# Where ScalarE makes the masks and the exponentials of a softmax round: masks ahead of the second turned tile, exponentials ahead of the last copy

## Time and profile before

| what | value |
|---|---|
| three runs | 974.4, 969.75, 970.98 us; median 970.98 |
| profiled execution | 970.57 us, span 969.0 us, granted clock 0.99 |
| TensorE busy | 908.8 us, 94% |
| VectorE busy | 717.8 us, 74% |
| GpSimd busy | 660.3 us, 68% |
| ScalarE busy | 577.4 us, 60% |
| chain that ended last | TensorE 71%, issue 10%, ScalarE 6%, VectorE 5%, GpSimd 3% |

### The profile page before, as it was taken

How to read it: one execution, slowest core, us unless ns; L and a number is a source line. 1 busy time by engine, 2 the same in 40 slices (tenths; PEclk the granted TensorE clock), 3 DMA queues, 4 the chain that set the end, 5 groups by cost and what they waited for, 6 DMA issues and landing times.

```text
span 969.0 us, 17781 instructions
## 1 busy us (share of the span) xinstructions
PE 908.8 (94%) x5132; PEld 690.2 (71%) x5133; DVE 717.8 (74%) x2191; ACT 577.4 (60%) x1226; POOL 660.3 (68%) x624
## 2 busy tenths in 40 slices
PE   4688999999999999999999999999999999999996
PEld 2354857768585776758586685957685998998895
DVE  5999999989999989999999899999503621251120
ACT  2577786777777777767777677776523321342211
POOL 7999997887988789888878879885453312231221
PEclk9999998999999999999999999999999999999998
DMA  5821121232211222121112222111043061116110
GB/s 196 253 58 46 42 59 57 58 113 55 60 44 56 68 58 67 44 68 51 49 58 57 63 58 60 53 30 46 13 145 100 18 221 56 54 38 222 43 54 32
DMA packets 69270, 70.84 MB, mean 73 GB/s; under 512 B 15456, under 2 KB 50560, under 8 KB 69184
## 3 DMA queue, kind: packets, MB, share of 16 engines
q1 hardware_dynamic: 65264, 59.44, 20.2%
q0 software_dynamic: 3920, 10.40, 3.5%
HBM read 59.05 MB, written 10.76 MB: 72 GB/s over the span
## 4 chain that ended last, share of the span: by engine, by line
PE 71%; issue 10%; ACT 6%; DVE 5%; POOL 3%; DMA 1%; POOLq 0%; SPq 0%; DVEq 0%; ACTq 0%
PE m_ps L1385 17%; PE m_ps L1467 10%; PE s_ps L1450 8%; PE t_ps L1342 7%; PE m_ps L1411 7%; PE o_ps L1358 5%; PE m_ps L1399 5%; PE s_ps L1324 4%; PE s_ps L1329 3%; PE o_ps L1450 3%; DVE top L1130 2%; ACT probs L927 1%; POOL dispatch_list L395 1%; PE m_ps L1418 1%; PE m_ps L1404 1%
## 5 line engine op out<-in xcount | busy, mean ns | idle before, releaser
L787 POOL TENSOR_TENSOR scores<-scores,below 128x576 f32<-128x576 f32 x144 | 200.3, 1417 | 88.0 <-ACT below L919 87.4
L1385 PE MATMUL m_ps<-xT,w_sb 128*128 128x192 f32 x1152 | 199.6, 331 | 1.2 <-ACT xT L963 1.2
L1385 PEld LDWEIGHTS m_ps<-xT,w_sb 128*128 128x128 f32 x1152 | 189.8, 193 | 1.5 <-ACT xT L963 1.5
L1130 DVE MAX8 top<-upper 128x8 f32<-128x288 f32 x384 | 159.4, 448 | 0.7 <-issue 0.6
L1132 DVE MATCH_REPLACE8 upper<-top,upper 128x288 f32<-128x288 f32 x288 | 125.3, 443 | 0.2 <-issue 0.2
L1342 PEld LDWEIGHTS t_ps<-ident,probs 128*128 128x128 f32 x720 | 80.3, 142 | 59.6 <-issue 51.1
L927 ACT ACTIVATE probs<-scores,shift 128x576 f32<-128x576 f32 x144 | 111.3, 783 | 18.3 <-issue 18.3
L956 ACT COPY probsT<-t_ps 128x640 f32<-128x640 f32 x192 | 103.4, 564 | 28.0 <-PE t_ps L1342 26.8
L1342 PE MATMUL t_ps<-ident,probs 128*128 128x128 f32 x720 | 107.4, 280 | 11.8 <-ACT probsT L956 11.8
L795 POOL TENSOR_SCALAR probs<-probs,inverse 128x576 f32<-128x576 f32 x144 | 105.4, 754 | 7.3 <-DVE inverse L1120 7.2
L919 ACT ACTIVATE below<-scores,steep_kth 128x576 f32<-128x576 f32 x144 | 106.6, 771 | 2.2
(11 more groups left out here) (208 smaller groups left out, 1789.1 us busy)
## 6 DMA issues: line engine op xcount, KB each, us to landing
k_sb<-keys_t SPq DMA_DIRECT2D x48, 288.0 KB, 2.6
v_sb<-values SPq DMA_DIRECT2D x48, 256.0 KB, 2.7
raw<-e_w SPq DMA_DIRECT2D x12, 1024.0 KB, 5.4
maxout_rows<-x_rows SPq DMA_DIRECT2D x18, 256.0 KB, 2.2
q_sb<-queries_t SPq DMA_DIRECT2D x48, 64.0 KB, 2.5
w_sb<-w SPq DMA_DIRECT2D x2, 1536.0 KB, 8.3
q_rest<-queries_t SPq DMA_DIRECT2D x96, 16.0 KB, 2.3
v_sb<-values SPq DMA_DIRECT2D x48, 32.0 KB, 2.6
```

Of the source, the lines that this page charges most:

```text
L787: nc.gpsimd.tensor_tensor(scores[:, r % RING, i, :], scores[:, r % RING, i, :], below[:, i, :], ALU.subtract).then_inc(masked_ready, 1)
L1130: nc.vector.max(best, src).then_inc(topk_step, 1)
L1385: ins = nc.tensor.matmul(dst[:, a * BLK:(a + 1) * BLK], w_sb[:, w, c, (first + a) * P:(first + a + 1) * P], xT[:, m % 2, c, b % SPAN * BLK ...
```

## The change

Only the places of ScalarE's steps change. `scalars` and all three `under` of round r stand at a new place, 5, ahead of H1 of round r. `exp(0)` and `exp(1)` of round r stand at place 9, ahead of the last M of round r. `exp(2)` of round r stands after Q0 of round r+1. Nothing is added or removed.

```diff
-AFTER_Q0, AFTER_H0, AFTER_H2, AHEAD_OF_LAST = 0, 3, 7, 9
+AFTER_Q0, AHEAD_OF_H1, AFTER_H2, AHEAD_OF_LAST = 0, 5, 7, 9
...
                 if in_range(r - 1):
-                    under_2, exp_0, exp_1, exp_2 = softmax_steps(r - 1)[3:]
-                    steps += [(AFTER_Q0, under_2), (AFTER_Q0, exp_0), (AFTER_H0, exp_1), (AFTER_H0, exp_2)]
+                    steps.append((AFTER_Q0, softmax_steps(r - 1)[6]))
+                if in_range(r):
+                    steps += [(AHEAD_OF_H1, step) for step in softmax_steps(r)[:4]]
...
                 if in_range(r):
-
-                    steps += [(AHEAD_OF_LAST, step) for step in softmax_steps(r)[:3]]
+                    steps += [(AHEAD_OF_LAST, step) for step in softmax_steps(r)[4:6]]
```

## The result

| kernel | runs | median | ratio to before | profiled execution | span | mean clock |
|---|---|---|---|---|---|---|
| before | 4 | 970.51 us | | 970.57 | 969.0 | 0.99 |
| changed | 4 | 1092.58 us (1087.77 to 1098.51) | 1.125, 95% interval [1.119, 1.132] | 1092.48 | 1090.9 | 0.956 |

What follows compares the result with a forecast made beforehand. The prediction took TensorE to set the pace, held up by waits for ScalarE's copies. To 970.6 us it added 91.2 of waits and 10 for the clock, giving 1071.8 us, stated as 1072, with a range of 1042 to 1112.

Steps and rivals of the forecast that it cites:

- TensorE sets the pace, and H1's copy is what it needs.: Masks ahead of H1's copy make TensorE's H2 start 2.24 us later in most rounds, 2.41 in parts 3 and 7.
- The exponentials ahead of the last copy.: Ahead of the last M copy: later copies make Q1 after parts 1 and 3 wait longer, +0.2 us per cycle.
- exp(2) early brings nothing but kth in time.: After the next round's Q0: VectorE's 1.08 us waits go without a gain in time, and kth comes sooner.
- `full_sum` with almost no wait: Sign on VectorE: its waits for the exponentials, 26.7 us in 25 rounds before, nearly vanish.
- Rival C: VectorE's kth comes too late for ScalarE, which stands with H1's copy; +42 us, 1114 us; chance 0.07.
- The first rounds.: Rounds 0 to 5: exponentials at the round's end hold back the next Q0 copy; +16.0 us at round 6.
- All waits.: Whole kernel: 16.0 to round 6, 12.7 in rounds 6 to 13, 58.0 in four cycles, 4.5 at the end; 91.2 us.
- The clock: From T of part 3 to L of part 4: a fall in all six cycles, four more than before, +10 us.
- I count none there: At the 2.24 us H2 waits of the A rounds: no clock falls, as a 0.87 us wait there had none.
- Rival A: The clock falls at A rounds' H2 waits too, in every second round; +45 us for the clock, 1107 us; chance 0.15.
- the main theory: Whole kernel: longer TensorE waits plus four more clock falls, 1072 us; chance 0.62.
- D, faster.: VectorE sets the pace, H2's wait vanishes in TensorE's slack and sums come sooner; 951 us; chance 0.03.

Runs made afterwards that it cites:

- experiment 3: The changed kernel with the masks one item later, behind H1's copy instead of ahead of it; 999.31 us, ratio 1.034 to before.
- Experiment 1: The changed kernel with four unused products filling TensorE's wait ahead of H2 wherever the first half does not end with Y; 1054.54 us, ratio 1.091 to before.
- experiment 2: The kernel before with only scalars and masks moved ahead of H1, the three exponentials left in their old places; 1123.76 us, ratio 1.161.
- experiments 4 and 5: The changed kernel with softmax rounds 0 to 5 in the old order, 1074.17 us; the same plus masks behind H1's copy, 984.04 us.
- experiments 6 and 7: The changed kernel with scalars and one mask, then two masks, ahead of H1's copy and the others behind it; 1011.19 us, then 1034.91 us.
- experiment 10: The kernel before: scalars, masks ahead of second half's first M; part 3's mask 1 after next Q0; part 2's last exponential behind H1's copy; 960.30 us.
- experiments 8 and 9: The kernel before with scalars and masks 0 and 1 ahead of the second half's first M, not its last, on two visits; 962.88 and 967.35 us.

## Why the prediction was right, and where it was short

- *TensorE sets the pace, and H1's copy is what it needs.* Right; experiment 3 shows it alone. The price was put at 2.24 us and is 2.16 (a wait of 2.07 in the timeline): from H1's copy to H2 it takes 0.81 us (383.52 to 384.33), not the 0.89 of the earlier trace rows. The waits in parts 3 and 7 are 2.17 (forecast 2.41), part 6 none. Part 2 waits 2.01 at H2, with the 0.42 at H1 gone, so it costs 0.6 more than before; forecast 0.5.
- *The exponentials ahead of the last copy.* Their own cost was forecast at +0.2 per cycle. Experiment 1, where the clock does not fall, shows Q1 waiting 0.45 and 0.72 us per cycle where it was 0.61 and 0.89: the change gives back 0.3 us here. (In the changed kernel itself the second of them is hidden, as V ran at the lower clock.)
- *exp(2) early brings nothing but kth in time.* Two things in this were wrong. The prediction let `full_sum` go earlier and named "`full_sum` with almost no wait" as a sign; it waits 132.6 us in place of 26.7, in nearly every round. In round 23 it stands for 4.14 us until exp(2) is done, behind a Q0 copy that comes later:

```profile
391.51 0.16 DVE L1115 TENSOR_REDUCE full_sum<-sums 128x3 f32<-128x6 f32 x1 [4.14 <-ACT probs L927]
```

VectorE has no more work than before, and the longer rounds leave it idle at this place. As TensorE sets the pace, this costs nothing. And "nothing" was too little: experiment 2 shows that with the exponentials left behind `kth` is late and the loss 35 us larger. Rival C was a real threat, which the other half of the change takes away. How the two halves hang together was in the prediction only as half a sentence.
- *The first rounds.* Forecast 16.0 us at Q1 of round 6. It stands at 114.22 in place of 97.16, 17.1 later, and Q2 of the same round at 121.26 in place of 105.70, 15.6 later. In this stretch the clock falls twice, which the sum did not have. Q1 of round 2 stands at 52.76, forecast 52.25. Taking the old order back there gains 14 and 15 us (experiments 4 and 5).
- *All waits.* Forecast +91.2 us, measured 75.9 + 7.4 = 83.3. The terms per round were a little high, as shown above. 4.0 of the 7.4 stand behind the attention rounds and are most likely not the change's (see Open). A cycle of eight rounds was forecast at 126.6 us and took 133.2, of which five falls are 8.5.
- *The clock* is the term that was mis-sized: forecast +10 us (four falls more), measured 37.7 by the windows and 34 by experiment 1. The step that failed is "I count none there" for the A rounds, taken from a wait of 0.87 us without a fall. That row was right for itself, and experiments 6 and 7 show the same at 0.74 and 1.40 us; but it was no row for a wait of 2.07. Rival A (a fall in every second lengthened round, 17 of them) came near the number of falls, 21 more than before; its price of 2.6 us was too high, since a fall costs 1.7 to 1.8 here. Its 1107 is 14 us above what was measured, the forecast 21 below: on the clock the rival was nearer than the main theory. That the forecast missed by only 21 us is in part luck, as its waits, 8 us too high, made up for some of the 28 us that the clock's term lacks.
- *D, faster.* Fell: VectorE's idle time grew instead. Its 95% occupancy did not mean that it set the pace.

Open: 4.0 us of TensorE's other waits stand at one place, 850 us, behind the attention rounds (a wait of L1404 for `stage`, with ScalarE's copies ahead of it late for no work that the trace names). A wait of 4.24 us at the same place is in the trace of experiment 10, and none in that of before. Of the two traces of the same kernel in experiments 8 and 9, one has it (4.26 us) and the other does not, so it comes and goes from execution to execution and is no sure effect of any placement. Its cause is open. The 2 us windows give the falls to 2 us, and one trace was looked at for each kernel.

## What to carry to other kernels

In an engine's in-order list, ask of each block which copy stands right behind it and how soon another engine needs that copy. Here the same masks cost 89 us more ahead of H1's copy than behind it. Where TensorE is the bound, a repeated pause costs more than its length once it makes the clock fall: look at the granted clock in the windows behind a pause as long as the one you are about to make, not behind a shorter one. And when a consumer is moved earlier (the masks), its producer's producers (the exponentials that `full_sum` waits for) have to move with it.

## What the runs showed of the hardware that was not expected

- The clock's falls do not grow evenly with the length of the pause: 3, 2, 4 and 24 falls in the whole kernel with waits of 0, 0.74, 1.40 and 2.07 us ahead of H2. At one and the same length of 2.0 to 2.2 us some waits are followed by a fall and some are not (16 of 38 in the changed kernel, 13 of 23 in experiment 2); all above 3 us are (2 of 2 and 18 of 18). Each fall cost 1.7 us in the cycle shown.
- Filling the pause with unused products took the falls away (24 to 3) and made the kernel 34 us faster with more work, 551.8 us of TensorE busy in 572 us in place of 502.3. The Trainium skill, "TensorE: Matmul & The Clock Gate", section "What's actually happening", has the clock follow how busy the engine has been; this pair of runs agrees.
